# Attention on one core: r turned as loaded and scaled out of PSUM, every turn on quarters of the array, the state's decay on GpSimd, and another order of the first units

## The reference

```python
    for t in range(S):
        kt, vt, rt = (k[:, :, t], v[:, :, t], r[:, :, t])
        cur = np.einsum('bhd,bhe->bhde', u[None] * kt, vt)
        y[:, :, t] = np.einsum('bhd,bhde->bhe', rt, state + cur)
        state = w[None, :, :, None] * state + np.einsum('bhd,bhe->bhde', kt, vt)
```

```python
    logits = x @ phi
    d = np.exp(logits - logits.max(0, keepdims=True))
    d /= d.sum(0, keepdims=True) + 1e-09
    slot_input = d.T @ x
...
        h = np.maximum(slot_input[e] @ w1[e], 0.0)
        slot_out[e] = h @ w2[e]
...
    return (c @ slot_out).astype(np.float32)
...
    h = x @ w_in
    g = np.where(h > 0.0, h, alpha * (np.exp(np.minimum(h, 0.0)) - 1.0))
    return (g @ w_out).astype(np.float32)
```

## Time and profile before

| | us |
|---|---|
| median of 3 runs | 409.14 |
| lowest and highest | 406.7, 409.24 |
| the profiled execution | 407.67 |
| its span in the trace | 405.5 |
| PE, DVE, ACT, POOL busy | 384.7, 275.8, 219.3, 114.7 |

### The profile page before, as it was taken

How to read it: one execution, slowest core, us unless ns; L and a number is a source line. 1 busy time by engine, 2 the same in 40 slices (tenths; PEclk the granted TensorE clock), 3 DMA queues, 4 the chain that set the end, 5 groups by cost and what they waited for, 6 DMA issues and landing times.

```text
span 405.5 us, 9559 instructions
## 1 busy us (share of the span) xinstructions
PE 384.7 (95%) x3528; PEld 341.6 (84%) x3528; DVE 275.8 (68%) x527; ACT 219.3 (54%) x502; POOL 114.7 (28%) x131
## 2 busy tenths in 40 slices
PE   6689999999998799988999999999999999999997
PEld 5588888888886435357999999999999999999996
DVE  4687777877765661079987677677676676776771
ACT  2676757676775214076655544645645465446441
POOL 4998778787870000037410000000000000000000
PEclk8999999999999999999999999999999999999999
DMA  6989899899987879970002000200100020002002
GB/s 128 184 241 259 161 265 267 190 234 270 240 251 290 305 291 423 401 222 18 0 2 78 2 0 2 78 0 0 45 33 0 0 78 0 0 0 78 2 0 78
DMA packets 84802, 51.84 MB, mean 128 GB/s; under 512 B 76704, under 2 KB 81952, under 8 KB 82336
## 3 DMA queue, kind: packets, MB, share of 16 engines
q1 hardware_dynamic: 84768, 51.37, 43.0%
HBM read 45.86 MB, written 4.72 MB: 125 GB/s over the span
## 4 chain that ended last, share of the span: by engine, by line
PE 87%; DVE 5%; issue 3%; POOL 3%; ACT 2%; DMA 0%; SPq 0%; DVEq 0%; POOLq 0%; ACTq 0%
PE psum L823 16%; PE psum L824 16%; PE psum L825 16%; PE psum L530 6%; PE psum L740 5%; PE psum L561 5%; PE psum L569 3%; PE psum L542 3%; PE psum L682 3%; PE psum L663 3%; PE psum L512 2%; PE psum L519 2%; PE psum L552 2%; PE psum L576 2%; PE psum L644 1%
## 5 line engine op out<-in xcount | busy, mean ns | idle before, releaser
L823 PE MATMUL psum<-w_out_hi,elu_hi 128*128 128x384 f32 x372 | 124.8, 336 | 1.3 <-DVE elu_lo L1063 1.3
L824 PE MATMUL psum<-w_out_lo,elu_hi 128*128 128x384 f32 x372 | 125.0, 336 | 0.0
L825 PE MATMUL psum<-w_out_hi,elu_lo 128*128 128x384 f32 x372 | 124.3, 334 | 0.0
L1214 ACT ACTIVATE exp_h<-psum 128x512 f32<-128x512 f32 x95 | 57.1, 601 | 97.3 <-PE psum L740 97.3
L1075 DVE SCALAR_TENSOR_TENSOR elu<-psum,neg_part 128x512 f32<-128x512 f32 x95 | 65.6, 691 | 56.8 <-ACT neg_part L1201 56.8
L824 PEld LDWEIGHTS psum<-w_out_lo,elu_hi 128*128 128x128 f32 x372 | 69.8, 188 | 3.6
L823 PEld LDWEIGHTS psum<-w_out_hi,elu_hi 128*128 128x128 f32 x372 | 69.8, 188 | 2.1 <-DVE elu_lo L1063 2.1
L1063 DVE TENSOR_TENSOR elu_lo<-elu,elu_hi 128x512 fp32r<-128x512 f32 x95 | 69.9, 735 | 0.1
L825 PEld LDWEIGHTS psum<-w_out_hi,elu_lo 128*128 128x128 f32 x372 | 69.9, 188 | 0.0
L1106 ACT ACTIVATE scores<-ident,bonus 128x128 f32<-128x128 f32 x192 | 58.7, 391 | 1.1 <-DVE bonus L874 1.1
L1201 ACT ACTIVATE neg_part<-exp_h 128x512 f32<-128x512 f32 x95 | 59.2, 624 | 0.1
(11 more groups left out here) (145 smaller groups left out, 428.3 us busy)
## 6 DMA issues: line engine op xcount, KB each, us to landing
w_sb<-in_moe_w_dram SPq DMA_DIRECT2D x8, 1536.0 KB, 7.9
w<-in_moe_w_dram SPq DMA_DIRECT2D x8, 1536.0 KB, 8.5
r_raw<-in_r_dram SPq DMA_DIRECT2D x24, 192.0 KB, 4.2
k_raw<-in_k_dram SPq DMA_DIRECT2D x24, 192.0 KB, 4.5
v_sb<-in_v_dram SPq DMA_DIRECT2D x24, 192.0 KB, 4.7
out_dram<-out_sb SPq DMA_DIRECT2D x24, 192.0 KB, 1.9
w_in_sb<-in_moe_w_in_dram SPq DMA_DIRECT2D x3, 1024.0 KB, 13.2
w_out_raw<-in_moe_w_out_dram SPq DMA_DIRECT2D x4, 768.0 KB, 12.2
```

The source lines that it names most:

```text
L823: pe.matmul(acc, hi, w_out_hi[:, f, :], start=(f == 0), stop=False)
L824: pe.matmul(acc, hi, w_out_lo[:, f, :], start=False, stop=False)
L825: m = pe.matmul(acc, lo, w_out_hi[:, f, :], start=False, stop=(f == KF2 - 1))
L1214: act.activation(exp_h[:, f % 2, :], banks[4 + f % RING][:, :], ACT.Exp).then_inc(exp_done, 1)
```

## The change

- r is no longer scaled before its turn. TensorE turns r as it was loaded, and VectorE multiplies by the table (now kept in turned form, tables_T) on the way out of PSUM: r_to_sbuf moves from ScalarE to VectorE and becomes a product. ScalarE gets the copy of the turned k in return. r_pair has three places.
- Every turn of r, k and x is written as 16 ordinary products with the identity, each on a quarter of the array: 64 tokens of one head, which are 48 columns of weights (64 for x) and 64 columns of identity (48 for x). r and k are turned into the same two banks. attend has half the keys in each product and twice as many products, so that it uses the same 64 by 64 tiles. key_values has 48 columns of weights in place of 64.
- GpSimd no longer makes r_nat; it makes k_nat, multiplies u and r into k's place (three units ahead; k_nat has three places), and does the state's decay.
- The order of each engine's work is another one (below); x and the logits share banks, which adds waits; w1 is loaded every fifth unit, and four loads of it in the last chunk.
- The first units: r and k of unit 0 and r of unit 1 are turned as loaded, VectorE scales the first two out of PSUM, only k_table is turned back, and GpSimd makes the products of units 0 and 1 first.
- At the end of attention turn_x of the last unit waits for the copy of logits_T and chunk_logits for the copy of x; slot_parts is copied in two halves.

```diff
+        ps_x = [banks[6][:, PAIRS * D:2 * PAIRS * D].rearrange("p (m e) -> p m e", m=PAIRS),
+                banks[7][:, 0:PAIRS * D].rearrange("p (m e) -> p m e", m=PAIRS)]
+        ps_x_both = psum[:, 6:8, :].rearrange("p k n -> p (k n)")[:, PAIRS * D:PAIRS * D + 2 * (BANK - PAIRS * D)].rearrange(
+            "p (r n) -> p r n", r=2)[:, :, 0:PAIRS * D]
...
-                    if un % KD == 1:
-                        load_w1(un // KD)
+                    if last:
+                        load_w1(E // 2 + b)
+                    elif un % 5 == 2:
+                        load_w1(un // 5)
                     if not last:
                         sp.wait_ge(bonus_ready, un + 1)
-                        sp.wait_ge(k_scaled, un + 1)
+                        sp.wait_ge(k_scaled, max(un + 1, 2))
+                        sp.wait_ge(r_turned, un + 1)
+                        sp.wait_ge(k_turned, un + 1)
                         load_rk(c + 1, b)
...
             sp.wait_ge(bonus_ready, UNITS)
+            sp.wait_ge(r_turned, UNITS)
+            load_w2(0)
             sp.wait_ge(kv_done, UNITS - B)
-            sp.wait_ge(r_turned, UNITS)
+            sp.wait_ge(state_ready, UNITS - B)
             sp.wait_ge(k_turned, UNITS)
-            load_w2(0)
+            sp.wait_ge(A_done, UNITS)
             load_w2(1)
             sp.wait_ge(y_done, UNITS)
             load_w2(2)
...
+            def k_to_nat(un):
+
+                pool.wait_ge(rk_loaded[un % B], 32 * (un // B + 1))
+                wait_for(pool, k_turned, un - 2)
+                wait_for(pool, kv_done, min(un - 2, UNITS - B))
+                pool.tensor_tensor(k_nat[:, un % 3], k_raw[:, un % B], k_table[:, :, :], ALU.mult).then_inc(k_scaled, 1)
+
+            def products(un):
+
+                b = un % B
+                pool.wait_ge(k_scaled, un + 1)
+                pool.tensor_tensor(k_raw[:, b], k_raw[:, b], u_row[:, :, :], ALU.mult).then_inc(ru_done, 1)
+                pool.wait_ge(ru_done, un + 1)
+                pool.tensor_tensor(k_raw[:, b], k_raw[:, b], r_raw[:, b], ALU.mult).then_inc(ruk_done, 1)
+
+
+            pool.wait_ge(u_loaded, 16)
+            for un in range(2):
+                pool.wait_ge(r_turned, un + 1)
+                pool.tensor_tensor(r_raw[:, un], r_raw[:, un], u_row[:, :, :], ALU.mult).then_inc(ru_done, 1)
+                pool.wait_ge(rk_loaded[un], 32)
+                pool.wait_ge(ru_done, un + 1)
+                pool.tensor_tensor(r_raw[:, un], r_raw[:, un], k_raw[:, un], ALU.mult).then_inc(ruk_done, 1)
+            pool.wait_ge(table_ready, 1)
+            pool.wait_ge(k_scaled, 1)
+            k_to_nat(0)
+            k_to_nat(2)
+            products(2)
...
+                    un = c * B + b
+                    if un + 3 < UNITS:
+                        k_to_nat(un + 3)
+                        products(un + 3)
+                    if not last:
+                        if first and b == 0:
+                            pool.wait_ge(powers, DECAY_SET)
+                        pool.wait_ge(state_summed, un + 1)
+                        if not first:
+                            pool.wait_ge(inter_done, un - B + 1)
+                        pool.tensor_tensor(state[:, b, :, 0:D], state_sum[:, :, :], decay[:, :, :], ALU.mult
+                                           ).then_inc(state_ready, 1)
...
+            def turn_quarters(turned, nat):
+
                 for a in range(PAIRS):
-                    m = pe.transpose((ps_A[n])[:, a, :], scores[:, 0, n * PAIRS + a, :], ident[:, :])
-                m.then_inc(tables_turned, 1)
-
-            def turn_r(un, i):
-                pe.wait_ge(r_scaled, un + 1)
-                wait_for(pe, r_ready, un)
-                for a in range(PAIRS):
-                    m = pe.transpose(ps_rT[:, a, :], r_nat[:, i, 2 * a:2 * a + 2, :], ident[:, :])
-                m.then_inc(r_turned, 1)
-
-            def turn_k(un, i):
-                pe.wait_ge(k_scaled, un + 1)
-                wait_for(pe, k_ready, un)
-                for a in range(PAIRS):
-                    m = pe.transpose(ps_kT[:, a, :], k_nat[:, i, 2 * a:2 * a + 2, :], ident[:, :])
-                m.then_inc(k_turned, 1)
-
-            def attend(un, i):
-
+                    for s in range(2):
+                        for two in range(2):
+                            rows = slice(s * HP, s * HP + HP)
+                            m = pe.matmul(turned[two * HP:two * HP + D, s, a, :], nat[rows, 2 * a + two, :],
+                                          ident[rows, rows], start=True, stop=True, skip_group_check=True)
+                return m
+
+            def turn_r(un):
+                pe.wait_ge(rk_loaded[un % B], 32 * (un // B + 1))
+                pe.wait_ge(k_ready, un + 1)
+                turn_quarters(ps_T, r_raw[:, un % B]).then_inc(r_turned, 1)
+
+            def turn_k(un):
+                pe.wait_ge(k_scaled, 1 if un == 1 else un + 1)
+                pe.wait_ge(r_ready, un)
+                if un == 2:
+                    pe.wait_ge(k_ready, 2)
+                turn_quarters(ps_T, k_nat[:, un % 3]).then_inc(k_turned, 1)
...
+                    for s in range(2):
+                        for two in range(2):
+                            rows = slice(two * HP, two * HP + D)
+                            keys = slice(s * HP, s * HP + HP)
+                            m = pe.matmul(ps_A[two][keys, a, :], k_pair[rows, i, a, keys], r_pair[rows, un % 3, a, :],
+                                          start=True, stop=True, skip_group_check=True)
                 m.then_inc(A_done, 1)
...
+                        m = pe.matmul(ps_kv[two * HP:two * HP + D, a, :], k_nat[:, un % 3, h, :],
+                                      v_sb[:, un % B, h, 0:D], start=True, stop=True, skip_group_check=True)
...
+            def turn_x(un):
+
                 pe.wait_ge(yT_ready, un + 1)
                 wait_for(pe, x_ready, un)
-                for a in range(PAIRS):
-                    m = pe.transpose(ps_x[:, a, :], y_T[:, a, b * P:(b + 1) * P], ident[:, :])
+                pe.wait_ge(state_summed, min(un + 2, UNITS - B))
+                for j in range(PAIRS):
+                    for s in range(2):
+                        for half in range(2):
+                            rows = slice(half * HP, half * HP + D)
+                            t0 = (un % B) * P + s * HP
+                            m = pe.matmul(ps_x[half][s * HP:s * HP + HP, j, :], y_T[rows, j, t0:t0 + HP],
+                                          ident[rows, rows], start=True, stop=True, skip_group_check=True)
                 m.then_inc(x_turned, 1)
...
+            pe.wait_ge(const_set, 4)
+            pe.wait_ge(rk_loaded[0], 32)
+            turn_quarters(ps_T, r_raw[:, 0]).then_inc(r_turned, 1)
+            turn_quarters(ps_T_A, k_raw[:, 0]).then_inc(k_turned, 1)
+            keep_clock_up_in(banks[5], 2)
+            pe.wait_ge(rk_loaded[1], 32)
+            turn_quarters(ps_T_x, r_raw[:, 1]).then_inc(r_turned, 1)
+            pe.wait_ge(tables_done, 2)
+            for a in range(PAIRS):
+                m = pe.transpose(banks[4][:, a * P:(a + 1) * P], tables_T[:, 1, a, :], ident[:, :])
+            m.then_inc(table_turned, 1)
+            keep_clock_up_in(banks[5], 2)
+            attend(0)
+            turn_k(1)
+            pe.wait_ge(r_ready, 2)
+            key_values(0)
...
+                    un = c * B + b
+                    if un + 2 < UNITS:
+                        turn_k(un + 2)
+                    if un + 1 < UNITS:
+                        attend(un + 1)
+                    if un + 2 < UNITS:
+                        turn_r(un + 2)
+                    if not first and b == 1:
+                        pe.wait_ge(lT_ready, c)
+                    if not first and b == 2:
+                        pe.wait_ge(logits_ready, c)
+                    if un >= 1:
+                        turn_x(un - 1)
                     if not first:
-                        state_in(un, b, i, c)
-                    if not (first and b == 0):
-                        turn_x(un - 1, (b - 1) % B)
+                        state_in(un)
+                    values(un, first)
+                    if un + 1 < UNITS - B:
+                        key_values(un + 1)
                     if not first and b == 0:
                         pe.wait_ge(phi_loaded, 64)
-                        if last:
-                            pe.wait_ge(state_summed, UNITS - B)
-                        else:
-                            pe.wait_ge(state_summed, un + 1)
+                        pe.wait_ge(x_ready, un)
+                        wait_for(pe, logits_ready, c - 1)
                         chunk_logits_T(c - 1)
                     if not first and b == 1:
-                        if not last:
-                            pe.wait_ge(state_summed, un + 1)
+                        pe.wait_ge(x_ready, un)
                         chunk_logits(c - 1)
...
```

(39 more changed lines are left out.)

242 lines of the change are left out of this document (76 added, 166 removed).

## The result

The changed kernel takes 457.95 us (median of 4 runs, 456.68 to 458.97) against 408.28 for the kernel before (406.70 to 409.24): a ratio of 1.122, with an interval of 1.116 to 1.128. It is 12% slower; 401.0 was forecast, and 407.5 was the end of the range. The profiled execution takes 458.87, its span 457.2.

The account below looks back on a forecast made before the run. The prediction took TensorE to bound attention, with DMA close behind. Gains of 2.5 + 6.6 + 0.5 less 1.5 made 8.1 us, so 399.6 for the profiled execution and 401.0 for the median; range 396.5 to 407.5.

Parts of the forecast that it names:

- 4.30 a unit: TensorE's time for one unit of attention, with 0.03 us added for waits; its pieces today sum to 4.63 us.
- step 2: Fourth attend to last attend: 98.4 us before, 91.8 after, a gain of 6.6 us.
- Rival A: Quarter turns on TensorE pass no faster than 27 ns a record, 0.87 us a turn: 431 us, slower; chance 0.12.
- Rival B: Another engine bounds attention at about 4.5 us a unit, through the ps_T loop or GpSimd: 405 us; chance 0.16.
- A turn's price: TensorE's time for a turn in quarters: 0.45 us for r, 0.46 for x, 0.64 for k with a shape change.
- The other pieces: TensorE's remaining groups in a unit: attend 0.88 us, state_in 0.44, values 1.02, key_values 0.38.
- two hand-overs of 0.05: From turn_k through ScalarE's copy to turn_r: hand-overs of 0.05 us each, in a loop of 1.33 us.
- Step 1: The start: fourth attend at about 23.5 us in place of 26.02, a gain of 2.5, between 0 and 4.
- Step 3: Last attend to last y copy, 6.38 us before: fewer shape changes and no added waits gain 0.5 us.
- Step 4: The tail to col_w: chunk_logits waits for x, a loss of 1.4 us, plus 0.1 for the slot_parts copy.
- Rival C: The start wins nothing because of a low clock and DMA's order: 403.5 us; chance counted within the forecast's own 0.62.
- Rival E: Turns on TensorE take an in-between time, 0.50 to 0.60 us: 405 to 412 us; chance 0.10.

Follow-up runs that it names:

- e_loop: The changed kernel with TensorE's attention as a hardware loop over chunks 1 to 4, other engines' programs as they are: 430.5 us.
- e_whole2: The changed kernel with whole 128x128 turns of r, k and x, the old tail, and ScalarE's k copy ahead of the logits' wait: 408.75 us, ratio 1.002.
- e_whole5: e_whole2 with w1 loaded in 24 pieces of 512 KB in place of 8 of 1.5 MB: 402.99 us, ratio 0.990.
- e_b_split: The kernel before with attend cut into 32 products and values into 16, same columns and nothing else changed: 433.88 us, ratio 1.066.
- e_w1_late: The changed kernel with all eight w1 loads in the last chunk: 445.9 us, ratio 1.094.
- e_b_fill: The kernel before with up to five more already reached waits ahead of each product and transpose of attention: 654.42 us.
- e_b_pieces: The kernel before with w1 loaded in 24 pieces of 512 KB, one a unit, in place of 8 of 1.5 MB: 406.81 us, ratio 1.001.

## Why the prediction was wrong

The step that failed is the forecast of TensorE's unit, "I add 0.03 for the waits: **4.30 a unit**", and with it step 2, "Gain 6.6": that stretch lost 50.3 us. In its place the runs showed a term that the sum has at nothing, the supply of instructions: pauses of 16.2 us in the 84 between 34 and 118 us, gone in the loop of e_loop. The prediction priced a turn in quarters by what 16 products take in the array and listed as risks the pace of records (A), another engine (B) and, as what it would have missed, a conflict in PSUM. It counted the records, "32 records where a transpose of a unit has four", and never asked how the engine gets them. "The engines that feed it" has r, k, the copies, GpSimd and DMA, and not the instruction queue, although the page of the kernel before lists one (q8, 23 packets). In that kernel's trace the two packets closest to each other start 3.86 us apart (39.92 and 43.78), where the forecast unit needed one in 3.0.

- **A turn's price** was right for x, 0.46 to 0.47 (0.46), and for k, 0.59 with a change of shape (0.64). The turn of r takes 0.58 where 0.45 was forecast: its 32 records begin over 0.45 us (104.80 to 105.25), but the first of them waits for ScalarE's copy of k. Rival A is refuted, since a turn's 32 records pass in 0.45 to 0.59 us, 14 to 18 ns each. The rule of the Trainium skill, "TensorE: Matmul & The Clock Gate", section "Wait — 56ns, not 53.3ns?", isn't a limit of the whole array: read so, it would make a turn 0.80, by the prediction's estimate.
- **The other pieces** held within 0.02: attend 0.88, state_in 0.45 (0.44), values 1.02, key_values 0.36 (0.38). What was mis-sized among them is the hand-over from the copy of k to the turn of r, "two hand-overs of 0.05": in the changed kernel the first weight load of turn_r comes 0.11 us after the copy's end in most units, and in the passes of e_loop 0.20 to 0.21, in its unrolled parts 0.11 again. So the hand-over itself is 0.06 over the forecast, and the loop adds 0.09. The turn of r takes 0.66 in e_loop, and the unit 4.45 against 4.30.
- **Step 1** gained 1.3 of 2.5 (24.76, 23.5 forecast, with two pauses of 0.6 to 0.8 before it); attend first ran at 11.34 (11.1). e_whole2, with the same new start and whole turns behind it, has its fourth attend at 23.85.
- **Step 3** can't be read: pauses lie in it.
- **Step 4** was right, and in its mechanism: the last turn of x begins 2.52 us after the last copy of y (2.51 forecast) and col_w 5.02 (5.01), a loss of 1.45 for 1.4.
- **Rivals B, C and E.** Rival B was a bound of another engine. In the changed kernel it can't be read, as every engine waits for TensorE; in e_whole5, another kernel, whose unit on TensorE is 4.31, DMA is at 1.01 and the gain is 4 us instead of 8. Rival C was a start that wins nothing: half of its gain came. Rival E, turns of 0.50 to 0.60, came true for the turn of r alone.

Had TensorE had its instructions, the units of e_loop say what was left: 0.17, 0.22 and 0.01 us gained (without and with the logits' two steps), 0.14 on average in place of 0.33, or 0.23 without the 0.09 of the loop. That is 2.9 to 4.6 us over 20 units for 6.6 forecast; with step 1 at 1.3 for 2.5 and steps 3 and 4 as forecast, the estimate is 404 to 406 us, 1% below before. So 3 to 5 of the 8.1 us that were forecast were there to gain, beside the 50 us of loss that it didn't see.

## What to carry to other kernels

Before cutting products into smaller ones, count instructions as well as array time: an fp32 product is two weight loads and two matmuls, a transpose one of each. In this kernel blocks of 256 instructions that last 7.6 us are free and those of 6.0 (e_whole2, 14 in 84 us) nearly so, with three pauses inside groups, 1.8 us in all; those that would last about 4.3 (e_b_split: some 290 a unit of 4.9 us) or 3.0 end in pauses of up to 3.1 and 4.5 us and a lower clock, the longest of them while a large load is under way. A pause inside a group, with every semaphore long reached, the same number of weight loads between two of them, and a packet of the instruction queue that lands some 1.4 us before the pause ends, is how it shows; a loop whose body stays in the engine removes it.

## What the runs showed of the hardware

- TensorE's supply: 11 packets in 84 us without a pause inside a group, 16 with (e_b_split), 18 in the changed kernel, 19 in e_w1_late. Between 34 and 118 us two packets start 3.8 us apart or more in the changed kernel and in e_w1_late, 3.3 in e_b_split, though one takes about 1.1 us; around loads of w1 the distance grows to 7.6 (7.9 in e_b_split). In e_w1_late, with no w1 in this stage, it stays below 5.8. Why packets keep that distance is open.
- All 89 pauses of more than 0.15 us between two records of one line, between 20 and 150 us in the traces of the changed kernel and of the runs other than e_b_fill, end 1.2 to 1.8 us after a packet of q8 has landed; the kernel before and e_b_pieces have none.
- A loop body of about 1,470 matmuls and weight loads (4 units of 352 and the logits' 66) stayed in the engine: no packet from 67.66 to 129.16 us over three passes.
- The four quarters of the array really run together: 16 products of 64x64 pass in 0.45 us.
- The granted clock falls to half behind some pauses (0.50 at 80.7 us, behind the one of 1.42 at 77.92), and in e_b_fill without a long one (0.57 between 34 and 60 us), when each pair of records was kept 0.3 us apart.
- Reached waits ahead of a product keep its weight load from starting early: in e_b_fill, where the trace has some three more wait instructions a product (3156 on TensorE against 180), the pairs of weight loads of key_values start 0.34 us apart, each load just ahead of its matmul, and the group takes 2.9 us for 0.45.
